# Fused attention and two MoE layers on one core: narrow products in two bursts per block, features by 32x32 squares from block 2, the last features' transfers ahead of the second expert weights

## The reference

```python
def _attn_ref(q, k, v, S1, S2):              # q, k, v: (4, 4, 1088, 32); S1, S2: (8, 32)
    phi(x): a = S1 x, b = S2 x (8 numbers each); all 64 products a_i * b_j
    q_p, k_p = (phi(q), phi(k))
    kv = np.einsum('bhsf,bhsd->bhfd', k_p, v); z = np.sum(k_p, axis=2)
    return (q_p kv) / (q_p z + 1e-6)
def _moe_ref(x, w_gate, w_val, w_out, rms_g):  # x: 4352 x 128, d_ff 1536
    xn = x / rms(x) * rms_g
    return silu(xn @ w_gate) * (xn @ w_val) @ w_out
def _moe2_ref(x, phi, w1, w2):               # 8 experts, 4 slots each, F 1024
    logits = x @ phi
    d = softmax of logits over tokens; slot_input = d.T @ x
    slot_out = max(slot_input @ w1, 0) @ w2, expert by expert
    return softmax of logits over slots @ slot_out
```

## Time and profile before

| | |
|---|---|
| median of 3 runs | 302.82 us (302.8 to 304.63) |
| the profiled execution: its time | 303.96 us |
| the profiled execution: its span, first to last instruction | 301.6 us |
| mean granted TensorE clock | 0.988 |
| PE, DVE, ACT, POOL busy | 95%, 76%, 53%, 10% of the span |

### The profile page before, as it was taken

One profiled execution on the slowest core, in us unless ns is written; L12 is line 12 of the kernel. 1 busy time (PEld: TensorE's weight loads), 2 busy tenths in 40 slices (PEclk: granted clock), 3 DMA queues, 4 the chain that ended last, 5 costly groups with the idle time before them and its releaser, 6 DMA issues.

```text
span 301.6 us, 6592 instructions
## 1 busy us (share of the span) xinstructions
PE 287.6 (95%) x2545; PEld 233.4 (77%) x2545; DVE 228.8 (76%) x440; ACT 159.5 (53%) x302; POOL 30.3 (10%) x50
## 2 busy tenths in 40 slices
PE   7789999999999989999999999999999999999983
PEld 6677787888787868888878788888788878797572
DVE  4747787976998797988788889797778668865423
ACT  1566654645566446346664473456446556547421
POOL 2087000000100010003100100020010003000000
PEclk9999999999999999999999999999999999999995
DMA  7999500000213123133112201982199311010016
GB/s 189 323 219 222 116 2 1 2 0 2 72 16 49 27 34 52 24 91 52 26 25 39 33 11 24 343 256 40 27 269 302 56 26 15 13 24 3 0 47 253
DMA packets 61040, 25.09 MB, mean 83 GB/s; under 512 B 45649, under 2 KB 57682, under 8 KB 61010
## 3 DMA queue, kind: packets, MB, share of 16 engines
q1 hardware_dynamic: 60722, 24.38, 33.5%
q10 hardware_dynamic: 288, 0.30, 0.3%
HBM read 17.45 MB, written 2.23 MB: 65 GB/s over the span
## 4 chain that ended last, share of the span: by engine, by line
PE 73%; DVE 12%; DMA 4%; issue 4%; ACT 3%; SPq 2%; DVEq 0%; ACTq 0%
PE bank L1006 70%; DMA area<-in_moe_w_out 4%; DVE hid L851 3%; DVE hl L857 3%; PE bank L1086 1%; ACT silu L578 1%; SPq L349 1%; DVE area L789 1%; DVE area L768 1%; DVE area L810 1%; DVE ssq L800 1%; DVE area L998 1%; PE bank L1047 1%; DVE area L744 0%; DVE area L759 0%
## 5 line engine op out<-in xcount | busy, mean ns | idle before, releaser
L851 DVE TENSOR_TENSOR hid<-bank,silu 128x512 f32<-128x512 f32 (+1 forms) x108 | 70.7, 655 | 42.7 <-ACT silu L578 20.8
L578 ACT ACTIVATE silu<-bank 128x512 f32<-128x512 f32 (+1 forms) x108 | 61.9, 573 | 70.9 <-PE bank L1006 70.2
L857 DVE TENSOR_TENSOR hl<-hid,hh 128x512 fp32r<-128x512 f32 (+1 forms) x108 | 71.2, 660 | 0.0
L586 ACT ACTIVATE hh<-hid 128x512 fp32r<-128x512 f32 (+1 forms) x108 | 64.9, 601 | 4.4 <-DVE hid L851 4.3
L1006 PE MATMUL bank<-xh,wgh 128*128 128x512 f32 (+1 forms) x108 | 42.4, 392 | 1.3 <-ACT xh L551 0.8
L1006 PE MATMUL bank<-hh,woh 128*128 128x512 f32 (+1 forms) x108 | 43.4, 402 | 0.0
L1006 PE MATMUL bank<-hh,wol 128*128 128x512 f32 (+1 forms) x108 | 41.1, 380 | 0.0
L1006 PE MATMUL bank<-xh,wvl 128*128 128x512 f32 (+1 forms) x108 | 41.1, 380 | 0.0
L1006 PE MATMUL bank<-xh,wgl 128*128 128x512 f32 (+1 forms) x108 | 41.0, 380 | 0.0
L1006 PE MATMUL bank<-xh,wvh 128*128 128x512 f32 (+1 forms) x108 | 41.0, 379 | 0.0
L1006 PE MATMUL bank<-hl,woh 128*128 128x512 f32 (+1 forms) x108 | 40.9, 379 | 0.0
(11 more groups left out here) (146 smaller groups left out, 336.2 us busy)
## 6 DMA issues: line engine op xcount, KB each, us to landing
area<-in_moe_w SPq DMA_DIRECT2D x1, 4096.0 KB, 14.5
area<-in_moe_w SPq DMA_DIRECT2D x8, 512.0 KB, 6.1
area<-area SPq DMA_DIRECT2D x96, 32.0 KB, 2.0
q_in<-in_q SPq DMA_DIRECT2D x16, 128.0 KB, 3.0
y_nat<-in_v SPq DMA_DIRECT2D x4, 512.0 KB, 6.3
out<-area SPq DMA_DIRECT2D x8, 256.0 KB, 2.5
area<-in_k SPq DMA_DIRECT2D x14, 128.0 KB, 5.7
y_nat<-area SPq DMA_DIRECT2D x112, 16.0 KB, 1.8
```

The costliest lines, as they stand in the source:

```text
L578: act.activation(silu[n][:, 0:w], gate_b[n][:, 0:w], ACT.Silu).then_inc(s_silu_ready, 1)
L586: act.activation(hh[m % NH][:, 0:w], hid[m % 2][:, 0:w], ACT.Copy).then_inc(s_hh_ready, 1)
L851: dve.tensor_tensor(hid[n][:, 0:w], val_b[n][:, 0:w], silu[n][:, 0:w], ALU.mult).then_inc(s_hid_ready, 1)
L857: dve.tensor_tensor(hl[m % NH][:, 0:w], hid[m % 2][:, 0:w], hh[m % NH][:, 0:w].bitcast(F32), ALU.subtract).then_inc(s_hl_ready, 1)
```

## The change

- NF goes from 3 to 2: block 2's features too are transposed by squares, and its `features_of(2)` stands in SP's queue ahead of the queries of batch 2.
- The projections of blocks 2 to 8 go from slot 1 (slot 8 for block 3) to slot 4, right behind the attention's products, and into `bank_c`, with waits to match. The key projections go from slot 9 to slot 7, right behind `normalised_T`, in banks 7 and 6.
- DVE's order is changed: `keys_T` in slots 1 to 3 (2, 5, 6 in block 0), `queries_T` in slot 0 or 3 (that of block 1 ahead of all slots), `mean_square` and `normalised` ahead of `step` of their slots, `features` in slot 5, `feature_squares` in slot 8 of every block, `finished_blocks` in slot 9 of every block.
- In SP's queue `features_of(8)` goes ahead of the wait and the loads of the second expert weights.

```diff
--- before.py
+++ after.py
@@ -104,7 +104,7 @@
         qp = area3[:, 0, :].rearrange("p (t f) -> p t f", t=HT)
 
 
-        NF = 3
+        NF = 2
         area5 = sb("area5", [P, 2 * HT * H * FT])
         qZ = area5[:, 0:HT * H * FT].rearrange("p (f n t u) -> p f n t u", n=HP, t=HT, u=NS)
         qpT = [x.rearrange("p (n w) -> p n w", n=HP) for x in (area3[:, 1, :], area5[:, HT * H * FT:])]
@@ -162,7 +162,11 @@
         assert M0 + HP * 2 * DA <= 512
 
         def kab_b(G):
-            return (bank[0:3] if G < NG else (bank_a, bank_b, bank_c))[G % NG]
+            return bank[G] if G < NG else psum[:, (7, 7, 6)[G % NG] * 512 + (0, AB * G3, 0)[G % NG]:][:, 0:AB * G3]
+
+
+        def ab_b(jn):
+            return bank_b if jn < NF else bank_c
 
         def mom_b(b):
 
@@ -402,8 +406,9 @@
                     by_head(q_in, q[b], h, s_q_loaded)
 
             load_queries(1)
+            features_of(NF)
             load_queries(2)
-            features_of(NF)
+            features_of(3)
             tokens_of(0)
             features_of(4)
             tokens_of(1)
@@ -417,13 +422,13 @@
             sp.dma_start(w1_sb, w1.rearrange("e d f -> d e f")).then_inc(s_w1_loaded, 16)
             features_of(7)
             tokens_of(4)
+            features_of(NB)
             sp.wait_ge(s_wg_lo, NG)
             sp.wait_ge(s_wv_lo, NG)
             sp.wait_ge(s_wo_lo, NG)
             for e in range(E):
                 sp.dma_start(w2_sb[:, e, :, :], w2[e].rearrange("(c p) d -> p c d", p=P)).then_inc(s_w2_loaded, 16)
 
-            features_of(NB)
             for j in range(5, NY):
                 tokens_of(j)
 
@@ -752,7 +757,7 @@
                 nt = width(jn) // P
                 if later(HP * jn) and jn <= NF:
                     dve.wait_ge(s_qpT_ps, HP * jn)
-                a_ij, b_j = factors(bank_b[:, 0:nt * H * NP * R], nt * H)
+                a_ij, b_j = factors(ab_b(jn)[:, 0:nt * H * NP * R], nt * H)
                 dve.wait_ge(s_ab_ps, jn + 1)
                 dve.tensor_copy(b_sb[:, 0:nt * H, :], b_j).then_inc(s_qb_ready, 1)
                 dve.wait_ge(s_qb_ready, jn + 1)
@@ -882,29 +887,28 @@
                         key_products(NG * keys_in(j - 1) + 2)
                     if c in (10, 11) and keys_in(j):
                         key_products(NG * keys_in(j) + c - 10)
-                    if c in (3, 6, 8) and keys_in(j):
-                        keys_T(NG * keys_in(j) + (3, 6, 8).index(c))
+                    key_c = (2, 5, 6) if first else (1, 2, 3)
+                    if c in key_c and keys_in(j):
+                        keys_T(NG * keys_in(j) + key_c.index(c))
                     if c == 2 and not first and keys_in(j - 1):
                         head_moments(keys_in(j - 1))
-                    if c == 0 and j + 1 < NF:
-                        queries_T(j + 1)
-                    if c == (5 if j + 2 == NF else 0) and NF <= j + 2 <= NB:
+                    if c == (0 if keys_in(j) and not first else 3) and NF <= j + 2 <= NB:
                         queries_T(j + 2)
-                    step(j, c)
-                    if c == 1 and j + 1 < NF:
-                        features(j + 1)
-                    if c == (8 if j + 2 == NF else 1) and NF <= j + 2 <= NB:
-                        features(j + 2)
-                    if c == (9 if j + 2 == NF else 6 if j + 2 == NF + 1 else 2 if keys_in(j) else 3) and NF <= j + 2 <= NB:
-                        feature_squares(j + 2)
-                    if c == (10 if j + 2 == NF else 9) and 0 <= j - 1 < NY:
-                        finished_blocks(j - 1)
-                    if c == 4 and not last:
-                        attention(j + 1)
                     if c == 5 and not last:
                         mean_square(j + 1)
                     if c == 6 and not last:
                         normalised(j + 1)
+                    if c == 1 and j + 1 < NF:
+                        features(j + 1)
+                    step(j, c)
+                    if c == 5 and NF <= j + 2 <= NB:
+                        features(j + 2)
+                    if c == 8 and NF <= j + 2 <= NB:
+                        feature_squares(j + 2)
+                    if c == 9 and 0 <= j - 1 < NY:
+                        finished_blocks(j - 1)
+                    if c == 4 and not last:
+                        attention(j + 1)
                     if c == 7 and not last:
                         split_x(j + 1, odd ^ 1)
                     if c == (2 if last else 6) and not first:
@@ -949,6 +953,8 @@
             mean_square(0)
             normalised(0)
             split_x(0, 0)
+            assert NF == 2
+            queries_T(1)
             whole_block(0, 0, 0, first=True)
             for b in range(1, B):
                 whole_block(b * 2 - 1, 1, b)
@@ -1027,15 +1033,17 @@
 
             def projections(jn):
                 pe.wait_ge(s_qT_ready, jn + 1)
-
-                ahead = 1 if jn > NF else 0
-                if later(2 * (jn - ahead)):
-                    pe.wait_ge(s_x_ready, 2 * (jn - ahead))
-                if later(jn - 2 - ahead):
-                    pe.wait_ge(s_logit_ready, jn - 2 - ahead)
+                if jn < NF:
+                    if later(2 * jn):
+                        pe.wait_ge(s_x_ready, 2 * jn)
+                elif jn == NF:
+                    pe.wait_ge(s_qpT_ready, HP * jn)
+                else:
+
+                    pe.wait_ge(s_qp_ready, jn)
                 for t in range(width(jn) // P):
                     for rows, tok in halves(t):
-                        ins = mm(bank_b[rows, t * AB:(t + 1) * AB], qT[:, tok], s_blk[:, :, :])
+                        ins = mm(ab_b(jn)[rows, t * AB:(t + 1) * AB], qT[:, tok], s_blk[:, :, :])
                 ins.then_inc(s_ab_ps, 1)
 
             def features_T(jn):
@@ -1054,8 +1062,6 @@
                     pe.wait_ge(s_qpT_ready, HP * jn + HP)
                 else:
                     pe.wait_ge(s_qZ_stored, FD * (jn + 1 - NF))
-                if NF <= jn < NB:
-                    pe.wait_ge(s_qp_ready, jn + 2)
                 pe.wait_ge(s_kv_ready, min(b + 1, B))
                 if later(jn - 1):
                     pe.wait_ge(s_yT_ready, jn - 1)
@@ -1149,9 +1155,11 @@
                     if G == 2:
                         pe.wait_ge(s_kTpads_ready, 1)
                     if b > 0 and G % NG == 0:
-                        pe.wait_ge(s_xl_ready, j + 2)
-                    if b > 0 and j > 0 and G % NG == 1:
-                        pe.wait_ge(s_logit_ready, j)
+                        pe.wait_ge(s_qp_ready, j + 3)
+                    if b > 0 and G % NG == 2:
+                        pe.wait_ge(s_x_ready, 2 * (j + 2))
+                        if j > 0:
+                            pe.wait_ge(s_logit_ready, j)
                     for t in range(G3):
                         for rows, tok in halves(G % NG * G3 + t):
                             ins = mm(kab_b(G)[rows, t * AB:(t + 1) * AB], kT[:, tok], s_blk[:, :, :])
@@ -1194,14 +1202,10 @@
                                 moments(keys_in(j - 1))
                             if j + 1 < NF:
                                 projections(j + 1)
-                            elif j + 2 <= NB:
-                                projections(j + 2)
-                        if c == 8 and j + 2 == NF:
-                            projections(j + 2)
-                        if c == 9 and keys_in(j):
-                            key_projections(keys_in(j), j)
                         if c == 4:
                             attention(j + 1, nb)
+                            if NF <= j + 2 <= NB:
+                                projections(j + 2)
                     if last and c >= C - 2:
 
                         pe.wait_ge(s_cshift_ready, NB)
@@ -1214,6 +1218,8 @@
                             features_T(j + 1)
                         if c == 7:
                             normalised_T(j + 1)
+                            if keys_in(j):
+                                key_projections(keys_in(j), j)
                     if c == 6 and j - 1 >= NY:
                         finish(j - 1)
                     if last and c == 1:
```

## The result

The changed kernel takes 308.12 us (median of 4 runs, 306.96 to 309.21), the kernel before 302.81 (4 runs): a ratio of 1.0148, 95% interval 1.0112 to 1.0184. The profiled execution has a span of 306.6 us and took 309.21.

What follows compares the result with a forecast made beforehand. The prediction took PE's stream as the bound; PE savings would be spent waiting on SP's queue, ending 4.0 us later, plus 1.5 for the clock: 302.82 + 4.0 + 1.5 = 308.3 us, range 304 to 312.5.

Steps and rivals of the forecast that it cites:

- VectorE's wait: Block 7, before `finished_blocks(6)`: VectorE stands 8.4 us until the transfers of `tokens_of(5)` land.
- The queue: SP's queue: `features_of(8)`, `w2`, `tokens_of(5)` in a row from 227.1 land at 262.1, making `finished_blocks(6)` 4.0 us later.
- `w2` does not shrink: SP's queue: the 4 MB of `w2` take 11.24 us because that is what the DMA engines move.
- The clock: Block 8: after PE's long wait its first products run at the lower clock level, adding 1.5 us (0 to 4).
- The savings: PE up to block 6, slot 8: 5.1 us less (4.0 to 6.3), 4.5 after a new 0.6 us wait.
- The fees of the projections: PE, blocks 3, 4, 6 and 8: projections lose the fee of a burst of their own, 4 x 0.36 = 1.44 us saved.
- `features_T(2)`: PE: this transpose burst goes, saving 0.88 us with the late start of the wide product behind it.
- the waits ahead of the transposes of blocks 2 and 4: PE before `normalised_T`: VectorE's new order removes 1.8 of 2.0 us of waits over all blocks.
- The 0.5 us for joining the keys to the transposes: PE, blocks 0, 2, 4: key projections behind the transposes save 0 to 0.36 us each, 0.5 in all.
- PE's wait ahead of `normalised_T(1)`: Block 0, with two `keys_T` lying in between: up to 0.4 us of PE's wait may stay.
- `features_of(7)` late by 0.6 us: SP's queue: the set lands at 214.3, wanted by the attention at 213.7, a new PE wait of 0.6 us (0 to 2.6).
- The first rival: SP's queue keeps up because sets of 16 transfers go out quickly; all PE savings stay, 297.3 us; chance 0.11.

Runs made afterwards that it cites:

- w2_behind_tokens5: The changed kernel with the loads of the second expert weights moved behind `tokens_of(5)` in SP's queue: 298.83 us, ratio 0.9841 to the kernel before.
- squares8_slot6: The changed kernel with the feature squares of block 8 made in slot 6 of block 6 instead of slot 8: 305.42 us, ratio 1.0073.
- w2_one_dma: The changed kernel with `w2` loaded by one DMA of 4 MB at the same place instead of eight of 512 KB: 307.65 us, ratio 1.0129.
- clock_kept_42: The changed kernel with 42 idle identity products on PE ahead of block 8's first gate product, to fill its wait: 307.46 us, ratio 1.0133.
- keys_own_burst: w2_behind_keys_early with the key projections of blocks 0, 2 and 4 behind slot 8's output, a burst of their own: 299.92 us, ratio 0.9903.
- w2_behind_keys_early: w2_behind_tokens5 with block 0's `keys_T` in slots 1, 2, 3 instead of 2, 5, 6: 299.54 us, ratio 0.9869.

## Why the prediction was right, step by step

The mechanism was right: a late start of `features_of(8)`, `w2` ahead of the tokens, VectorE's wait, PE's wait, the clock. That the sum comes within 0.2 us of the median is luck. The chain came 0.7 us less late than forecast, what follows it cost 0.3 more, and the four runs alone lie 2.3 us apart.

- **The queue** held term by term from `features_of(8)` on. Its squares were ready: 227.1 forecast, 227.26 measured; its transfers 10.4 and 10.40; `w2` 11.24 and 11.24; `tokens_of(5)` 11.3 and 10.5 (249.06 to 259.57); landing 1.8 and 1.85; `finished_blocks(6)` 262.2 and 261.51. VectorE's wait was 8.4 forecast, 7.55 measured. The two sets before it became ready later than forecast (`features_of(6)` 170.89 instead of 168.7, `features_of(7)` 200.80 instead of 199.9), and it made no difference, since a hole stood behind each. That the wait is for these transfers and that it sets the end is shown by w2_behind_tokens5 and squares8_slot6.
- **`w2` does not shrink**: right in what matters, since one DMA holds the queue as long as eight do (w2_one_dma). Not exact: the eight took 11.0 to 11.2 us to issue in four traces and 10.0 to 10.2 in six, so about 1 us of the 11.24 was not fixed. What decides between the two is open.
- **The clock**: 1.5 us forecast; 2.3 by block 8 in clock_kept_42, 2.4 beside the kernel before. Only 1.8 of it shows in the span, since the tail was 0.6 us shorter in this execution.
- **The savings** up to block 6, slot 8, 4.5 us forecast, look right with 4.3 but were made of other terms. 0.95 us of them is a start that came early in this one profile (first gate product at 21.34; 22.29 before, 21.6 to 22.5 in the other traces). Counted from the first gate product, slot 8 of block 6 comes after 205.5 us in both traces of the old order of work and after 199.9 to 202.1 in the nine of the new one: 3.4 to 5.6 us saved, and this profile is one of the two with 3.4. The fees of the projections and `features_T(2)` went as counted. So did the waits ahead of the transposes of blocks 2 and 4, which by the gaps around them were worth 2.0 us and not the 1.55 of the rows. The 0.5 us for joining the keys to the transposes is 0 (keys_own_burst), and these two errors nearly cancel. And block 0 lost instead of gaining: VectorE waits 2.8 us for the queries of batch 1, `projections(2)` makes PE wait 0.3 us, and PE's wait ahead of `normalised_T(1)` is 0.9 us where the forecast left 0.4. That the queries' load had no time in hand was overlooked. How much it costs depends on the execution: VectorE's wait for them is 2.4 to 2.8 us in the two traces that start earliest and 0 to 1.2 in the other seven, and PE's wait behind it is then 0.3 at most.
- **`features_of(7)` late by 0.6 us**: it was not, at 11.60 us of issuing instead of 12.5; it was late by 0.9 in w2_behind_keys_early, with 12.39, and by 1.0 in w2_one_dma, with 12.19. The margin there is nil, as argued.
- **The first rival**, that the queue keeps up, was wrong as a forecast, but its time (297.3) is near what the kernel reaches when the queue does: 298.8. The section of the Trainium skill on which the rival leaned (DMA: Bandwidth & Descriptors, Anatomy of one DMA) describes DMAs that GpSimd issues. Here SP issues them, and each of the quick ones takes it 0.60 to 0.62 us, so that section gave no ground for short sets.

## What to carry to other kernels

An engine that issues transfers in program order is a resource with a length of its own, even if the DMA engines are a fifth busy. Before moving the work that makes a set of transfers ready, lay out that queue to its end: slack that is burnt as a hole early on comes back as a wait at the last set, behind whatever bulk load stands between. A bulk load goes where nothing behind it in the queue is urgent. And work saved ahead of a wait is not saved: the engine only stands longer, and if it is PE it may then start again at half its clock, so that the kernel ends later than before.

## What the runs showed of the hardware

- One 4 MB DMA issued in 0.82 us holds back the next DMA of the same queue for 11.44 us when that one stands right behind it; eight of 512 KB take 10.0 to 11.2 us to issue. Either way the bulk load holds the queue for most of the time that the data take (the 4 MB of `w1` landed 13.0 to 15.5 us after they were issued).
- 16 transfers of 16 or 32 KB between parts of SBUF take 10.2 to 12.4 us to issue when no bulk load is under way, at some 0.60 us each in the quickest sets; the DMA engines are then mostly idle (share 0.17 and 25 GB/s for the 16 KB ones, 0.32 and 49 GB/s for the 32 KB ones).
- The granted clock fell in PE waits of 3.9, 4.7, 7.9 and 7.97 us, and in 2.6 us of standing behind 7.3 us of dense products; it did not in waits of up to 1.3 us. One such fall cost block 8 about 2.3 us.
- A burst of 64-column products has a fee of 0.36 us between two wide products (an estimate from bursts of 16 and of 36). The fee is saved when the burst joins the attention's products (1.67 and 0.81 us apart, 2.13 together) and is still paid behind 128x128 transposes (0.44 and 1.40 us apart, 1.84 together).
- Of the tokens' transfers most land in 1.8 us, beside a busy PE too; single ones took up to 4.2. In the two runs with PE busy in the wait, the last of the set, for which VectorE waits, was such a one (3.76 and 3.81 us, otherwise 1.83 to 1.85). The cause was not tried.
